# Loading each expert matrix of a mixture-of-experts kernel in four transfers instead of one

## The chip, the cores and the metric

The kernel runs on one core of a Trainium2 chip. The metric is the device time of one execution in microseconds (us), lower is better.

## The reference

Three layers run one after the other, all in float32:

```python
def reference(**kwargs):
    attn_out = _attn_ref(q, k, v)                      # 4 x 8 heads x 576 x 64, causal window of 64
    x = attn_out.transpose(0, 2, 1, 3).reshape(2304, 512)
    x = _moe_ref(x=x, w_skip, w_gate, w1, w2)
    return _moe2_ref(x=x, w_in, w_out)                 # 512 -> 2048, hard swish, 2048 -> 512

def _moe_ref(x, w_skip, w_gate, w1, w2):
    out = x.copy()
    xc = x[x @ w_skip > 0]
    logits = xc @ w_gate
    e_idx = np.argmax(logits, axis=1)
    for e in range(8):
        mask = e_idx == e
        h = np.maximum(xc[mask] @ w1[e], 0.0)          # w1[e]: 512 x 1024, 2 MB
        y[mask] = gate_w[mask, None] * (h @ w2[e])     # w2[e]: 1024 x 512, 2 MB
    out[do_compute] = xc + y
    return out
```

About half of the 2304 tokens are skipped; each of the others goes through one of eight experts.

## The kernel before

The instruction streams of the engines are written by hand and ordered by semaphores. There are three stages.

**Attention and routing** (to about 120 us). Eighteen blocks of 128 tokens are loaded, scored, and scattered by GpSimd (L696) to rows of a DRAM table, `x_rows`, so that the tokens of an expert stand together.

**Experts** (about 120 to 273 us). The tokens of each expert are worked on in tiles of 64; the number of tiles of an expert is read from a table at run time, so each engine has one hardware loop per expert. In this execution there are 17 tiles for the eight experts. For one tile TensorE makes the first product from `w1s` (L994, 128 matmuls), turns the tokens of the next tile around (L965, two transposes of `xin`), and makes the second product from `w2s` (L1006, 32 matmuls). ScalarE applies the relu, two chunks of the hidden layer at a time, to `hT` (L1245, four instructions for a tile), and copies the turned tokens to `xeT` (L1210). L1006 begins only when the first of the four `hT` instructions of its tile is done. VectorE forms the output `yo` (L1700), and GpSimd stores it to `x_rows` (L758). SyncE loads the tokens of a later tile to `xin`, in two transfers of 65 KB (L541), as soon as the two transposes of the one before have freed `xin`.

**Last layer** (about 273 us to the end). Six blocks at a time go through the 512 to 2048 to 512 layer (L1035, L1093), with weights that SyncE loads in small pieces (L548, L550, L556).

**The expert matrices.** There are three pairs of buffers, `w1s[e % 3]` and `w2s[e % 3]`, each with a semaphore of its own. The helpers `load_w1` (L321) and `load_w2` (L324) issue one transfer of 2 MB each, and `wait_w1` (L328) and `wait_w2` (L332) are TensorE's waits, the first at the head of an expert's loop, the second ahead of L1006 in each tile. SyncE loads expert 0 after the attention loads (L535), and expert 2 (L586) between the tiles of experts 0 and 1. ScalarE loads expert 1 after the first tile, and then, at the end of expert e, expert e + 3 into the pair that has come free (L1270, L1271), before it enters the loop of expert e + 1:

```python
                if e + 3 < NE:
                    sc.wait_ge(s_y, end)
                    fixed(sc)
                    load_w1(sc, e + 3, s_wp1[e % 3])
                    load_w2(sc, e + 3, s_wp2[e % 3])
```

Here `s_y` says that the last L1006 of expert e is done. ScalarE issues its own transfers in its own stream, so while it issues one it applies no relu. Below, "crossing e" is the time from the end of the last L1006 of expert e to the first L1006 of expert e + 1. Five crossings carry a load: those after experts 0 to 4.

Of the kernel before, what the change touches and what calls it, by code (L numbers as in the profile page):

```python
# [5 lines left out]
def attention_moe_mlp_kernel(nc, q, k, v, moe_w_skip, moe_w_gate, moe_w1, moe_w2,  # L6
# [20 lines left out]
    P = 128  # L27
# [10 lines left out]
    DC = DM // P  # L38
    FC = F // P
# [21 lines left out]
    with ctx:  # L61
# [3 lines left out]
        def sem(name):  # L65
            return ctx.enter_context(nc.semaphore(name))
# [19 lines left out]
        w1s, w2s = [], []  # L86
# [168 lines left out]
        s_wp1 = [sem(f"s_wp1_{i}") for i in range(3)]  # L255
        s_wp2 = [sem(f"s_wp2_{i}") for i in range(3)]
# [45 lines left out]
        SEQ = [LEAD] + list(range(LEAD)) + list(range(LEAD + 1, NE))  # L302
# [15 lines left out]
            eng.sem_inc(s_step, 1)  # L318

        def load_w1(eng, e, signal):  # L320
            eng.dma_start(w1s[e % 3][:, :, :], moe_w1[SEQ[e]].rearrange("(c p) f -> p c f", p=P)).then_inc(signal, 16)  # L321

        def load_w2(eng, e, signal):
            eng.dma_start(w2s[e % 3][:, :, :], moe_w2[SEQ[e]].rearrange("(c p) f -> p c f", p=P)).then_inc(signal, 16)  # L324

        def wait_w1(eng, e):

            eng.wait_ge(s_wp1[e % 3], 16 * (e // 3 + 1))  # L328

        def wait_w2(eng, e):  # L330

            eng.wait_ge(s_wp2[e % 3], 16 * (e // 3 + 1))  # L332

        def lg_bank(T):

# [174 lines left out]
        def _(sp):  # L510
# [20 lines left out]
            for T in range(1, NT):  # L531
                for n in loads_of(T):
                    load_qk(n)
                load_v(T)
            load_w1(sp, 0, s_wp1[0])  # L535
            load_w2(sp, 0, s_wp2[0])

            def load_rows(row):
# [35 lines left out]
            for e, first, end in expert_tiles(sp, first_bounds(sp)):  # L574
                base = R0 + e * R
                if e == 0:
                    with sp.Fori(0, end - 1) as t:
                        sp.wait_ge(s_ready, t + later + 1)
                        fixed(sp)
                        sp.wait_ge(s_xet, t + 1 + XT0)  # L580
                        sp.wait_ge(s_xmid, t + 1 + XM0)
                        load_rows(bass.ds(t * ET + (base + ET), ET))
                    continue
                if e == 1:
                    sp.wait_ge(s_ready, 2 * RD0)
                    load_w1(sp, 2, s_wp1[2])  # L586
                    load_w2(sp, 2, s_wp2[2])
                elif e == 2:
                    sp.wait_ge(s_padp, 16 * (NE - 2))
                elif e == 4:  # L590
                    load_w_in(0)
                elif e == 5:
                    load_w_out(0)
                    load_w_in(1)
                elif e == 7:
                    load_w_out(1)
                with sp.Fori(0, end - first) as t:
                    g = first + t
                    row = t * ET + base
                    sp.wait_ge(s_xet, g + XT0)  # L600
                    sp.wait_ge(s_xmid, g + XM0)
                    load_rows(bass.ds(row, ET))
# [174 lines left out]
        def _(pe):  # L777
# [203 lines left out]
            for e, first, end in expert_tiles(pe, bounds):  # L981
                wait_w1(pe, e)
                fixed(pe)
                with pe.Fori(0, end - first) as t:
                    g = first + t
                    pe.wait_ge(s_xetc, g + 1)
                    for m in range(FC // 2):

                        pe.wait_ge(s_hc, g * (FC // 2) + m - 4 + HC0 + 1)
                        for f in range(2 * m, 2 * m + 2):  # L990
                            for c in range(DC):
                                for x in range(2):
                                    cols = f * P + x * W
                                    last = pe.matmul(bank[m % 4][x * W:(x + 1) * W, (f % 2) * ET:(f % 2 + 1) * ET],  # L994
                                                     w1s[e % 3][:, c, cols:cols + W],
                                                     xeT[:, c % 2, c // 2, :], start=(c == 0), stop=(c == DC - 1))
                        last.then_inc(s_h, 1)
                    pe.wait_ge(s_xin, g * 32 + 64)
                    transpose_x()
                    wait_w2(pe, e)  # L1000
                    pe.wait_ge(s_yc, g + YC0)
                    for f in range(FC):
                        if f % 2 == 0:
                            pe.wait_ge(s_hc, g * (FC // 2) + f // 2 + HC0 + 1)
                        for x in range(2):
                            last = pe.matmul(bank[6][x * ET:(x + 1) * ET, 0:DH], hT[:, f, :],  # L1006
                                             w2s[e % 3][:, f, x * DH:(x + 1) * DH],
                                             start=(f == 0), stop=(f == FC - 1))
                    last.then_inc(s_y, 1)
# [115 lines left out]
        def _(sc):  # L1125
# [124 lines left out]
            for e, first, end in expert_tiles(sc, bounds):  # L1250
                if e == 0:
                    tile_of_expert(0)
                    sc.wait_ge(s_xin, 32 * 3)
                    load_w1(sc, 1, s_wp1[1])
                    load_w2(sc, 1, s_wp2[1])
                    first = 1
                with sc.Fori(0, end - first) as t:
                    tile_of_expert(first + t)
                if e == 4:
                    w_high(0)  # L1260
                    w_rest_high(0)
                elif e == 5:
                    o_high(0)
                elif e == 6:
                    w_high(1)
                    w_rest_high(1)
# [5 lines that stand above are left out]
# [605 lines left out]
```

## Time and profile before

| | |
|---|---|
| median of 3 runs | 666.27 us (664.95 to 668.8) |
| span of the profiled execution | 667.5 us |
| time of the profiled execution around its span | not listed; the span alone is |
| TensorE busy | 632.4 us, 95% of the span |
| ScalarE busy | 321.5 us, 48% |
| mean granted TensorE clock | 0.990 |
| bytes read and written in DRAM | 80.08 MB and 12.97 MB |
| the expert matrices among them | 16 transfers of 2048 KB |

The profile covers one execution. Its page gives the busy time of each engine and the chain of work that ended last. The chain is followed back from the last instruction: at each step it names what released the step. The timeline lists instructions by start and duration; issuing a transfer shows as a piece on the queue of its engine (SPq, ACTq), and the time to landing is counted from that issue to the last semaphore update.

### The profile page before, as it was taken

The page shows a single profiled execution, that of the slowest core. Times are in us where ns is not written, and L with a number is a line of the kernel's source. Part 1 is how long each engine was busy: PE and PEld are TensorE (multiplying, and loading weights), DVE is VectorE, ACT ScalarE, POOL GpSimd, SP SyncE. Part 2 cuts the span into 40 slices and gives each one's busy share as a digit, 9 for nine tenths or more (in the row PEclk, how much of TensorE's full clock was granted, in tenths as well). Part 3 has the DMA queues.
Part 4 walks back from the last instruction along what each step waited for, and adds up shares of the span by engine and source line. Part 5 has one row for each costly group of instructions (what it writes and reads, how often), then busy time and mean ns, then how long its engine had stood idle before and what let it go on. Part 6 is the DMA issues. An engine that isn't in the chain of part 4 may idle for free.

```text
span 667.5 us, 17127 instructions
## 1 busy us (share of the span) xinstructions
PE 632.4 (95%) x6454; PEld 549.9 (82%) x6454; DVE 396.2 (59%) x1070; ACT 321.5 (48%) x674; POOL 91.6 (14%) x160
## 2 busy tenths in 40 slices
PE   7899986798799989999999999999999999999998
PEld 6688874676678868898898898888888988888896
DVE  2678886311111122497766679777777788777743
ACT  3798884111112122664454556654455475444433
POOL 4333452431101011100000002100000021000000
PEclk9999999799989999999999999999999999999999
DMA  9876848498878785622222222623222233122102
GB/s 157 179 175 151 204 125 329 135 326 282 274 288 307 241 313 186 198 64 80 79 80 64 63 64 66 205 79 80 80 63 64 64 110 111 64 63 64 33 0 95
DMA packets 114132, 93.56 MB, mean 140 GB/s; under 512 B 62893, under 2 KB 90033, under 8 KB 114065
## 3 DMA queue, kind: packets, MB, share of 16 engines
q1 hardware_dynamic: 97696, 56.10, 30.9%
q10 hardware_dynamic: 12720, 25.58, 11.0%
q0 software_dynamic: 3648, 11.00, 4.4%
q8 instruction: 41, 0.67, 0.4%
q14 instruction: 27, 0.21, 0.1%
HBM read 80.08 MB, written 12.97 MB: 139 GB/s over the span
## 4 chain that ended last, share of the span: by engine, by line
PE 84%; DMA 4%; DVE 4%; issue 3%; ACT 1%; POOLq 1%; another core or an unknown queue 1%; POOL 0%; SPq 0%; DVEq 0%
PE bank L1093 30%; PE av L1035 27%; PE bank L994 7%; PE av L1006 7%; DMA xin<-x_rows 3%; PE bank L807 2%; PE av L851 2%; PE bank L792 2%; PE bank L867 2%; DVE sm L1460 1%; DMA x_rows<-yo,yrow 1%; PE av L965 1%; PE bank L897 1%; PE av L1022 1%
## 5 line engine op out<-in xcount | busy, mean ns | idle before, releaser
L1093 PE MATMUL bank<-o_hi,g_lo 128*128 128x512 f32 x288 | 114.0, 396 | 0.0
L1093 PE MATMUL bank<-o_hi,g_hi 128*128 128x512 f32 x288 | 113.9, 395 | 0.0
L1093 PE MATMUL bank<-o_lo,g_hi 128*128 128x512 f32 x288 | 113.5, 394 | 0.0
L1035 PE MATMUL av<-xc_hi,w_hi 128*128 128x384 f32 x344 | 89.5, 341 | 0.0
L1035 PE MATMUL av<-xc_hi,w_lo 128*128 128x384 f32 x344 | 88.3, 337 | 0.0
L1035 PE MATMUL av<-xc_lo,w_hi 128*128 128x384 f32 x344 | 88.2, 337 | 0.0
L1764 DVE TENSOR_TENSOR g_lo<-act,g_hi 128x384 fp32r<-128x384 f32 x96 | 53.4, 556 | 43.6 <-ACT g_hi L1328 40.4
L994 PEld LDWEIGHTS bank<-xeT,w1s 128*64 128x64 f32 x2176 | 69.2, 139 | 10.7 <-issue 8.4
L994 PE MATMUL bank<-xeT,w1s 128*64 128x64 f32 x2176 | 71.1, 224 | 6.4 <-issue 5.9
L1328 ACT CAST g_hi<-act 128x384 fp32r<-128x384 f32 x96 | 49.4, 515 | 51.4 <-DVE act L1757 49.4
L1035 PEld LDWEIGHTS av<-xc_hi,w_hi 128*128 128x128 f32 x344 | 63.0, 188 | 13.2 <-DVE act L1757 0.9
L1245 ACT ACTIVATE hT<-bank 128x128 f32<-128x128 f32 x68 | 18.8, 278 | 114.4 <-PE bank L994 108.4
L1318 ACT ACTIVATE rel<-hq,half 128x384 f32<-128x384 f32 x60 | 37.0, 617 | 70.4 <-DVE hq L1750 70.4
L1093 PEld LDWEIGHTS bank<-o_hi,g_lo 128*128 128x128 f32 x288 | 54.0, 188 | 13.0
L1006 PE MATMUL av<-w2s,hT 128*64 128x256 f32 x544 | 63.2, 385 | 0.3 <-DVE yo L1700 0.3
L1035 PEld LDWEIGHTS av<-xc_lo,w_hi 128*128 128x128 f32 x344 | 62.6, 188 | 0.0
L1035 PEld LDWEIGHTS av<-xc_hi,w_lo 128*128 128x128 f32 x344 | 62.4, 188 | 0.0
L1093 PEld LDWEIGHTS bank<-o_lo,g_hi 128*128 128x128 f32 x288 | 54.3, 188 | 6.5
L1093 PEld LDWEIGHTS bank<-o_hi,g_hi 128*128 128x128 f32 x288 | 54.0, 188 | 6.2
L1006 PEld LDWEIGHTS av<-w2s,hT 128*64 128x64 f32 x544 | 38.0, 138 | 20.8 <-issue 3.1
L1694 DVE COPY yo<-xres 128x4 f32<-128x4 f32 x17 | 2.9, 170 | 74.2 <-DMA x_rows<-yo,yrow 70.3
L1138 ACT ACTIVATE pr<-sm,mx 128x128 f32<-128x128 f32 x144 | 45.7, 396 | 1.4 <-DVE mx L1460 1.2
(182 smaller groups left out, 945.0 us busy)
## 6 DMA issues: line engine op xcount, KB each, us to landing
w1s<-in_moe_w ACTq DMA_DIRECT2D x6, 2048.0 KB, 10.1
w2s<-in_moe_w ACTq DMA_DIRECT2D x6, 2048.0 KB, 17.1
wor<-in_moe_w_out SPq DMA_DIRECT2D x24, 512.0 KB, 3.8
wir<-in_moe_w_in SPq DMA_DIRECT2D x24, 256.0 KB, 4.2
wir<-in_moe_w_in SPq DMA_DIRECT2D x48, 128.0 KB, 4.1
qraw<-in_q SPq DMA_DIRECT2D x36, 128.0 KB
vnow<-in_v SPq DMA_DIRECT2D x36, 128.0 KB, 3.6
kraw<-in_k SPq DMA_DIRECT2D x34, 128.0 KB
```

The source lines that it names most:

```text
L792: last = pe.transpose(dst[:, pi * P:(pi + 1) * P], src[:, 2 * pi:2 * pi + 2, :].rearrange("p h d -> p (h d)"), ident[:, :])
L807: last = pe.matmul(bank[2 + p][x * W:(x + 1) * W, j * KH:(j + 1) * KH], qT[T % 3][rows, j, x * W:(x + 1) * W], kT[T % 3][rows, j, 0:3:2, : ...
L851: last = pe.matmul(av[x * W:(x + 1) * W, h // HP, at0:at0 + VW], prT[T % 2][:, h, x * W:(x + 1) * W], (vnow if x else vprev)[:, T % 3, h, ...
L994: last = pe.matmul(bank[m % 4][x * W:(x + 1) * W, (f % 2) * ET:(f % 2 + 1) * ET], w1s[e % 3][:, c, cols:cols + W], xeT[:, c % 2, c // 2, : ...
L1006: last = pe.matmul(bank[6][x * ET:(x + 1) * ET, 0:DH], hT[:, f, :], w2s[e % 3][:, f, x * DH:(x + 1) * DH], start=(f == 0), stop=(f == FC - 1))
L1035: last = pe.matmul(into[:, 0:GN], a[it % 2][:, W_AT[w], c, :], b[:, X_AT[x], c, :], start=(n == 0 and fresh), stop=(n == 3 * XQ * len(pair ...
L1093: last = pe.matmul(bank[tile][:, :], a[c][:, i * P:(i + 1) * P], b[it % 2][:, units(it)[c], :], start=(p == 0 and c in (0, 2) and n == 0), ...
L1138: last = sc.activation(pr[T % 2][:, h, :], sm[:, h, :], ACT.Exp, scale=-1.0, bias=mx[T % 2][:, h:h + 1])
L1245: sc.activation(hT[:, 2 * m:2 * m + 2, :], bank[m % 4][:, 0:2 * ET].rearrange("p (f s) -> p f s", f=2), ACT.Relu).then_inc(s_hc, 1)
L1318: sc.activation(rel[n % 2][:, :], quarter(it, c), ACT.Relu, scale=1.0 / 6.0, bias=half[:, :]).then_inc(s_rel, 1)
L1328: sc.copy(g_hi[c][:, :], act[n % 2][:, :]).then_inc(s_ghi, 1)
L1764: dve.tensor_tensor(g_lo[c][:, :], act[n % 2][:, :], g_hi[c][:, :].bitcast(fp32), ALU.subtract).then_inc(s_glo, 1)
```

## The change

`load_w1` issues four transfers, one for each 128 rows of the matrix, and `load_w2` four, one for each two chunks of 128 rows. All four add to the semaphore that the one transfer added to, and the two waits ask for four times the count. Where the loads stand in the streams, the buffers and the bytes are as before.

```diff
         def load_w1(eng, e, signal):
-            eng.dma_start(w1s[e % 3][:, :, :], moe_w1[SEQ[e]].rearrange("(c p) f -> p c f", p=P)).then_inc(signal, 16)
+            for c in range(DC):
+                eng.dma_start(w1s[e % 3][:, c, :], moe_w1[SEQ[e], c * P:(c + 1) * P, :]).then_inc(signal, 16)
 
         def load_w2(eng, e, signal):
-            eng.dma_start(w2s[e % 3][:, :, :], moe_w2[SEQ[e]].rearrange("(c p) f -> p c f", p=P)).then_inc(signal, 16)
+            rows = moe_w2[SEQ[e]].rearrange("(c p) f -> p c f", p=P)
+            for c in range(0, FC, 2):
+                eng.dma_start(w2s[e % 3][:, c:c + 2, :], rows[:, c:c + 2, :]).then_inc(signal, 16)
 
         def wait_w1(eng, e):
 
-            eng.wait_ge(s_wp1[e % 3], 16 * (e // 3 + 1))
+            eng.wait_ge(s_wp1[e % 3], 16 * DC * (e // 3 + 1))
 
         def wait_w2(eng, e):
 
-            eng.wait_ge(s_wp2[e % 3], 16 * (e // 3 + 1))
+            eng.wait_ge(s_wp2[e % 3], 16 * (FC // 2) * (e // 3 + 1))
```

Here DC is 4 and FC is 8.

## Rows read from the trace of the kernel before

**Rows 1.** The page: its head, and the chain that ended last, by engine.

```profile
span 667.5 us, 17127 instructions
PE 84%; DMA 4%; DVE 4%; issue 3%; ACT 1%; POOLq 1%; another core or an unknown queue 1%; POOL 0%; SPq 0%; DVEq 0%
```

**Rows 2.** The chain in order of time, expert stage (start us, us, what).

```profile
155.91 9.37 DMA xin<-x_rows
...
165.76 3.60 PE av L1006 x32
...
173.92 3.60 PE av L1006 x32
...
180.20 3.42 issue
...
186.12 4.32 PE av L1006 x32
...
198.46 2.67 PE bank L994 x91
...
203.01 3.60 PE av L1006 x32
...
226.85 0.38 PE av L965 x2
...
228.10 7.72 DMA xin<-x_rows
...
264.83 2.73 PE bank L994 x93
```

**Rows 3.** Issue to landing of the 2 MB transfers, L321 and then L324.

```profile
DMA to landing us min/median/max: 8.8/10.1/14.1
...
DMA to landing us min/median/max: 14.5/17.0/20.0
```

**Rows 4.** Timeline of ScalarE at crossings (start us, us, engine line op out<-in).

```profile
169.92 1.09 ACTq L324 DMA_DIRECT2D w2s<-in_moe_w  x1
171.75 0.28 ACT L1245 ACTIVATE hT<-bank 128x128 f32<-128x128 f32 x1 [5.58 <-issue]
...
178.06 0.75 ACTq L324 DMA_DIRECT2D w2s<-in_moe_w  x1
...
198.59 0.37 ACTq L321 DMA_DIRECT2D w1s<-in_moe_w  x1
198.99 0.53 ACTq L324 DMA_DIRECT2D w2s<-in_moe_w  x1
200.29 0.28 ACT L1245 ACTIVATE hT<-bank 128x128 f32<-128x128 f32 x1 [5.02 <-PE bank L994]
...
224.57 0.28 ACT L1245 ACTIVATE hT<-bank 128x128 f32<-128x128 f32 x1 [5.12 <-PE bank L994]
```

**Rows 5.** Lines L556 and L635: what issuing one takes (ns min/median/max).

```profile
L556 SPq DMA_DIRECT2D wor<-in_moe_w_out x24: 367/368/506, 221.2 to 616.8; - x24
...
L635 SPq DMA_DIRECT2D out<-ot x3: 332/351/360, 661.4 to 662.8; - x3
```

**Rows 6.** Timeline of SyncE: the load of expert 2, and a run of small loads.

```profile
150.40 0.51 SPq L324 DMA_DIRECT2D w2s<-in_moe_w  x1
155.24 11.87 SPq L541 DMA_DIRECT2D xin<-x_rows  x4
...
262.52 1.44 SPq L616 DMA_DIRECT2D xn<-x_rows  x3
264.01 1.39 SPq L616 DMA_DIRECT2D x_first<-x_rows  x3
...
267.93 0.51 SPq L556 DMA_DIRECT2D wor<-in_moe_w_out  x1
```

**Rows 7.** Issue to landing of `wor` (512 KB), and of `x_first` (260 KB each).

```profile
DMA to landing us min/median/max: 3.6/3.8/8.3
...
DMA to landing us min/median/max: 5.4/5.5/5.7
```

## The prediction, made before the kernel was run

> **What bounds the kernel now.** I read the page first, then the chain in order of time, then the timeline of the two engines that issue the loads. TensorE carries 84% of the chain that ended last, DMA 4% and "issue" 3% [rows 1]. The change touches the transfers of the expert stage alone, so the question is where that stage has a gap that a weight load makes. The chain shows three large ones [rows 2]. From 155.91 it waits 9.37 us for `xin`. That transfer was issued on SyncE's queue behind the 4 MB of expert 2, issued there to 150.91 [rows 6]. From 228.10 it waits 7.72 us for `xin` again, while the matrices of expert 6 are in flight, though these are on ScalarE's queue; most of that lies beside TensorE's work: a tile takes 8.16 us from L1006 to L1006 (165.76 to 173.92), so after the L1006 of 227.23 the next was due at 235.4, and it began after 235.82 + 0.44 = 236.3. And from 180.20 TensorE stands 3.42 us in the middle of the first tile of expert 2 with nothing it waited for ("issue"). The L1006 after it takes 4.32 us instead of 3.60.
>
> No gap is a wait for the matrices themselves. A load is issued almost two experts ahead. The shortest cover is expert 7: its `w2` is issued by about 241, the slowest of the six took 20.0 us to land [rows 3], so 261, and its first L994 begins at 264.83 [rows 2]. So nothing is gained by matrices that arrive sooner, and the new waits ask for all four pieces anyway.
>
> **The change, part by part.**
>
> *Waits with four times the count.* The same number of instructions, and they are satisfied when the last piece is in, as before. Nothing; the cover is the 3.8 us just worked out for expert 7. If the eight pieces took over 3.8 us longer, that expert would wait.
>
> *Issue on SyncE, experts 0 and 2.* Two issues become eight. For one quarter of `w2` there is a row with the same shape, 2 x 128 pieces of 2 KB: `wor`, 0.37 us, 0.51 at most. For a quarter of `w1` (128 contiguous rows) the nearest is `out`, 0.33 to 0.36 us [rows 5]; I take 0.36. With 0.03 us between two issues, eight take 4 x 0.39 + 4 x 0.40 = 3.2 us, against 0.38 + 0.03 + 0.51 = 0.92 us. So SyncE comes free 2.2 us later. For expert 2 that is 153.2 instead of 150.9. What is queued behind is the load of `xin`, which does not go out before 155.24 [rows 6], since `xin` is not free sooner. Hidden, with 2 us to spare. For expert 0 SyncE has nothing else to issue for about ten microseconds.
>
> *Issue on ScalarE, experts 1 and 3 to 7.* This is the term that can show. Expert 1 is loaded early in a tile, with the relus all behind it and over 4 us of TensorE's L994 ahead of the L1006 that needs them: hidden. At the five crossings the budget is tighter. At crossing 2, L1006 ends at 198.46; ScalarE issues `w1` from 198.59, `w2` to 199.52, spends 0.77 us on entering the next loop, and runs its first `hT` at 200.29, done at 200.57. TensorE asks for that `hT` at 203.01 [rows 2, 4]. The slack is 2.44 us and the added issue time 2.2 us: hidden, by 0.2 us. Crossing 3: `hT` done at 224.85, asked for at 226.85 + 0.38 = 227.23, slack 2.38: hidden, by 0.2 us. Crossing 0: the `w2` issue took 1.09 us there, `hT` was done at 172.03, asked for at 173.92, slack 1.89: 0.3 us late. Crossing 1: the 3.42 us stop puts the next L1006 at 186.12, so all is hidden. Crossing 4 has the same steps as crossing 2. The three later `hT` come 0.3 us apart and are asked for every 0.9 us, so only the first counts. Sum: +0.3 us, say +0.4 with the signal. Lower bound 0. Upper bound: all eight cost what the dearest similar issue did, 0.51 to 0.53 us plus 0.03, so 4.5 us, 3.5 more than before: 1.6 late at crossing 0, and 1.1 at each of 2, 3 and 4, or 4.9 us in all.
>
> *The transfers themselves.* The bytes, the row sizes and the engine that moves them are unchanged; only the order of rows within `w1` differs, and each piece ends with a completion of its own, six more per expert. No row has a piece boundary alone. The nearest is the run of three `xn` and three `x_first` from 262.52: the last is issued at about 264.97 and landed 5.7 us later, so six loads of 260 KB took 8.15 us [rows 6, 7]. The same 1.56 MB at the rate of a 2 MB load that follows another (2 MB in the 17.0 - 10.1 = 6.9 us between the landings of `w1` and `w2` [rows 3]) is 5.2 us, plus 1.3 us at the start as an estimate from 3.8 us for the 512 KB of `wor` (1.7 us of data, the rest split between start and completion). That leaves 1.65 us for five boundaries, 0.3 each at most, and other traffic ran beside it. Six more boundaries are at most 2.0 us per expert. Hidden wherever the matrices have cover; on the path once, at expert 2, since `xin` waits behind them (9.37 us). I take 0, since the pieces follow in one queue without a wait. Bounds: below, -1 us, should contiguous rows of `w1` be read faster; above, +2.0 us.
>
> The sum against the profiled execution is 667.5 + 0.4 = 667.9 us. Its span is 1.2 us above the median of the runs, so on the median: 666.3 + 0.4 = **666.7 us**. A measurement of this kernel can tell about 0.5%, 3.3 us, from no change.
>
> **The rivals.**
>
> *A. The issues hold ScalarE (slower).* An issue may wait when many transfers are outstanding on its queue. For it: 0.75 us at 178.06, while the load of expert 3 was still in flight, against 0.53 us [rows 4]. Against it: at 267.93 SyncE issued `wor` in 0.51 us with three `x_first` (landing 5.5 us after 264 to 265) and three `wir` outstanding, six in all [rows 6, 7]. With eight issues, the eighth has seven ahead of it, and at crossing 1 eleven. It decides from the point where the first `hT` is done later than 4.55 us after the last L1006. If the eighth has to wait for the first piece to land (3.8 us, as `wor`), ScalarE is free at 4.3, `hT` done at 5.3 us: 0.8 us late at four crossings; at crossing 1, where it would have to wait for expert 3 to land at about 187, some 2 us after the stop. With the tail of such waits, +3 to +8 us: 669 to 674 us, 672 as its middle.
>
> *B. Each piece pays its own start and end (slower).* If pieces went one after another, each would take the 3.8 us of `wor`: 30 us instead of the 17.4 for the pair, 13 us more, on the path at `xin` behind expert 2, and about 5 us at expert 7, past its cover: 666.3 + 13 + 5 = 684 us. Against it: the six loads above, 1.36 us each where a lone 512 KB takes 3.8.
> The Trainium skill (DMA: Bandwidth & Descriptors, "Anatomy of one DMA" and "Rules for kernel authors") puts a fixed cost of some 2.0 us on one DMA (stated for GpSimd's path) and asks for 1 MiB or more in each. Six more of these per expert would be 12 us if they added up; the trace of six loads in 8.15 us speaks against their adding up.
>
> *C. Small transfers get their turn sooner (faster).* If what stops TensorE at 180.20, and `xin` at 228.10, is waiting behind long runs of a big transfer, shorter ones may let them in sooner. All of it would be 3.42 + 0.72 us and about 1 us, some 5 us: 661.5 us; a share of it is likelier. Against it: the pieces stand in the queue one right behind the other, as the one transfer did.
>
> *D. The change does not do what it says.* Issues in the trace are counted per transfer, so four per matrix will show; nothing merges them. I give it nothing of its own.
>
> **How the numbers follow.** Forecast (hidden, but for tenths) 0.74; A 0.13; B 0.04; C 0.09. The forecast's own range is 664.5 to 669.5. The range for all, with the bounds of the ScalarE term (+4.9) and half of A, is 663.5 to 671.5. Faster by over 0.5% (below 663.0): half of C and a little of run to run change, 0.07. Slower by over 0.5% (above 669.6): B, most of A, and the upper end of the issue term, 0.17. Within 0.5%: 0.76.
>
> **What would show it.** In the profile of the changed kernel: 24 issues of `w1s` and 24 of `w2s` on ACTq of 512 KB each, 0.35 to 0.40 us apiece; the first `hT` after a crossing some 4.0 us after the end of L1006, not 1.8; L1006 to L1006 over a crossing unchanged at 8.15 us or up by a few tenths. SyncE's `xin` after expert 2 still issued near 155.2 and landing near 165.3. `w1s` complete at about 10 us and `w2s` at about 17 us after the first issue. It is wrong if an issue on ACTq takes over 0.6 us in the median (A), if `xin` after expert 2 lands several us later (B), or if the stop at 180.20 is gone (C).

## The result, and the profile after

The changed kernel takes 676.4 us (median of 4 runs, 674.33 to 679.82), against 666.46 us for the kernel before. The ratio is 1.0138, with a 95% interval of 1.0095 to 1.0181: 1.4% slower. The profiled execution took 674.66 us; its span is 673.0 us, 5.5 us above that of the profile before. It is one of the two quicker runs of the four, and the profile before is that of the slowest run of its kernel (668.8 us), so the two profiles show about half of the loss.

The page of the changed kernel, its head and the chain that ended last:

```profile
span 673.0 us, 17175 instructions
PE 86%; DVE 4%; ACTq 3%; issue 2%; DMA 2%; ACT 2%; another core or an unknown queue 1%; SPq 0%; DVEq 0%
```

ACTq, ScalarE's issuing of transfers, is on the chain now with 3%; before it had no share at all [rows 1]. DMA went down from 4% to 2%. So the chain does not wait for transfers to move, but for an engine to issue them. The chain in order of time, at crossing 2 (start us, us, what; L1009 is the L1006 of before, L997 the L994, L1248 the L1245):

```profile
195.35 3.63 PE av L1009 x32
...
199.08 0.35 ACTq L322
...
199.46 0.46 ACTq L322
...
199.94 0.46 ACTq L322
...
200.43 0.62 ACTq L322
...
201.08 0.48 ACTq L327
...
201.59 0.54 ACTq L327
...
202.16 1.49 ACTq L327
...
203.68 0.73 ACTq L327
...
205.18 0.29 ACT hT L1248
...
205.51 1.08 PE av L1009 x7
```

From L1009 to L1009 it is 10.16 us here; before it was 8.15 us (194.86 in the trace of before, to 203.01 [rows 2]). The eight issues took 5.33 us, from 199.08 to 204.41, where the prediction had put 3.2 us. Their durations over the whole kernel (ns min/median/max):

```profile
L322 ACTq DMA_DIRECT2D w1s<-in_moe_w x24: 352/455/1431, 133.8 to 246.6; - x24
L322 SPq DMA_DIRECT2D w1s<-in_moe_w x8: 348/434/621, 95.9 to 151.0; - x8
...
L327 ACTq DMA_DIRECT2D w2s<-in_moe_w x24: 455/573/1575, 135.6 to 248.7; - x24
L327 SPq DMA_DIRECT2D w2s<-in_moe_w x8: 469/662/846, 98.0 to 153.7; - x8
```

The piece of `w2` has the shape of `wor`, which took 367/368/506 ns [rows 5], and the median here is 573 ns on ScalarE. Only the first issue of `w1` in a run takes 0.35 to 0.38 us; those right behind it take 0.45 us and more.

The waits of the expert stage (engine, line, waited for: us in total, times, longest):

```profile
PEld av L1009 <- ACT hT L1248: 7.9, 5, 2.3
...
PE av L1009 <- ACT hT L1248: 6.6, 4, 2.0
```

TensorE waits 6.6 us for `hT`, four times; before, only the weight load showed such a wait, 0.9 us in total. From the L1006 at the start of crossing 0 to the last one it was 103.58 us before (165.76 to 269.34) and is 109.45 us now (165.43 to 274.88), 5.9 us more. By the same starts the crossings 0 to 4 took 8.16, 12.20, 8.15, 8.19 and 8.75 us before and 10.14, 11.58, 10.16, 9.92 and 8.97 us now: 5.3 us more. Crossing 1 hides it in this run, since there an "issue" stop stood in both kernels, 3.42 us before and 1.92 us now.

At the other four the prediction's own sum, filled with what was measured, gives the loss (us; the time held runs from the start of the first issue to the end of the last):

| crossing | held before | held now | added | slack before | added less slack | crossing longer by |
|---|---|---|---|---|---|---|
| 0 | 1.51 | 5.33 | 3.82 | 1.89 | 1.93 | 1.98 |
| 2 | 0.93 | 5.33 | 4.40 | 2.44 | 1.96 | 2.01 |
| 3 | 1.03 | 5.09 | 4.06 | 2.38 | 1.68 | 1.73 |
| 4 | 0.94 | 4.15 | 3.21 | 3.03 | 0.18 | 0.22 |

The load of expert 2 on SyncE cost nothing here: its eight issues ran from 149.66 to 154.22, 4.56 us, and `xin` behind them was issued at 155.03. It is waited for from 155.90 for 9.06 us; before it was 155.91 and 9.37 us [rows 2].

### The profile page after: what moved, and what is told of

Same layout as the page of the kernel before. It is cut to its first block, busy times and chain, and to the rows that moved or that the text cites. A ratio compares the mean times of both kernels' runs of the same rounds, so it can differ in the third digit from the quotient of the medians.

```text
span 673.0 us, 17175 instructions
## 1 busy us (share of the span) xinstructions
PE 635.3 (94%) x6454; PEld 551.0 (82%) x6454; DVE 396.2 (59%) x1070; ACT 319.6 (47%) x674; POOL 91.1 (14%) x160
## 4 chain that ended last, share of the span: by engine, by line
PE 86%; DVE 4%; ACTq 3%; issue 2%; DMA 2%; ACT 2%; another core or an unknown queue 1%; SPq 0%; DVEq 0%
PE bank L1096 30%; PE av L1038 27%; PE av L1009 9%; PE bank L997 7%; PE bank L810 2%; PE av L854 2%; PE bank L795 2%; PE bank L870 2%; ACTq L327 2%; DVE sm L1463 1%; DMA xin<-x_rows 1%; ACTq L322 1%; PE av L968 1%; PE bank L900 1%
## 5 line engine op out<-in xcount | busy, mean ns | idle before, releaser
L997 PEld LDWEIGHTS bank<-xeT,w1s 128*64 128x64 f32 x2176 | 69.8, 140 | 9.5 <-issue 7.2
L997 PE MATMUL bank<-xeT,w1s 128*64 128x64 f32 x2176 | 72.2, 225 | 4.7 <-issue 4.0
L1248 ACT ACTIVATE hT<-bank 128x128 f32<-128x128 f32 x68 | 17.2, 279 | 123.7 <-PE bank L997 95.3
L1009 PE MATMUL av<-w2s,hT 128*64 128x256 f32 x544 | 64.3, 390 | 7.1 <-ACT hT L1248 6.6
L1009 PEld LDWEIGHTS av<-w2s,hT 128*64 128x64 f32 x544 | 38.4, 140 | 28.6 <-ACT hT L1248 7.9
```

The lines of the kernel that those rows point to most:

```text
L1248: sc.activation(hT[:, 2 * m:2 * m + 2, :], bank[m % 4][:, 0:2 * ET].rearrange("p (f s) -> p f s", f=2), ACT.Relu).then_inc(s_hc, 1)
```

## The experiments

The runs were made on several chips, on which the kernel before takes 652 to 668 us, so each is compared with runs of the kernel before on the same chip. Lines are numbered anew in each kernel.

**1. Which engine's pieces cost.** Only ScalarE's loads cut in four:

```diff
+        def parts1(e):
+            return 1 if e in (0, 2) else 4
```

> Only the loads that ScalarE issues (experts 1 and 3 to 7) are cut in four; SyncE's two (experts 0 and 2) are one transfer of 2 MB each again. Theory I (the extra issues hold ScalarE at the crossings): as slow as the changed kernel, 8 to 11 us above before. Rival T (the small pieces slow the transfers, and what waits behind them): the xin behind expert 2 is as before, so part of the loss comes back, by 2 us or more.

Measured: 670.08 against 652.69 us, ratio 1.0262 (1.0194 to 1.033). The loss is there, and it is larger than the 1.4% of the first chip; the changed kernel itself did not run on this one. In the profile TensorE's matmuls wait 10.8 us for `hT`, in place of 6.6, and two of the second products (the L1006 of before) behind such waits, at 229.74 and 248.62, take 5.07 and 5.36 us in place of 3.60. The slack is smaller on this chip too: with ScalarE's loads whole (the next run) crossings 0, 2 and 3 take 7.7 us from L1006 to L1006, against 8.15 to 8.19 us on the first chip.

Only SyncE's loads cut in four (`return 4 if e in (0, 2) else 1`):

> Only SyncE's loads (experts 0 and 2) are cut in four. Theory I: as before, within 1.5 us, since SyncE has time to spare. Rival T: slower by 2 us or more, with xin landing after 165.8 us in the chain where before it landed at 165.3.

Measured: 656.49 against 652.69 us, ratio 1.0035 (0.9992 to 1.0079), not to be told from no change, though 5 us is not excluded: in its profile the chain runs through SyncE's eight issues (141.38 to 146.09) to the `xin` behind them. Most of the loss, at the least, lies where ScalarE issues the pieces.

**2. Issues without the pieces.** The matrices whole, and six tiny transfers behind them at each crossing:

```diff
                     load_w2(sc, e + 3, s_wp2[e % 3])
+                    for n in range(6 * e, 6 * e + 6):
+                        sc.dma_start(lgs[n // 15][:, n % 15 * 8:n % 15 * 8 + 8], moe_w2[0, 0:P, n * 8:n * 8 + 8]).then_inc(s_tiny, 16)
```

> The matrices are loaded in transfers of 2 MB as before, and at each of the five crossings ScalarE issues six more transfers of 4 KB in all (128 rows of 32 bytes) to a tile that nothing reads. Theory I: slower by 5 to 11 us, like the changed kernel, with the first relu after a crossing 5 to 6 us after the last L1006 in place of 2. Rival T: within 1.5 us of before, as the big transfers are whole.

Measured: 698.74 against 652.69 us, ratio 1.0717 (1.0639 to 1.0795). The sign was right, and the loss of 46 us over four times the largest that was expected. The issues (ns min/median/max), and ScalarE's timeline at crossing 1:

```profile
L1275 ACTq DMA_DIRECT2D lgs<-in_moe_w x30: 505/772/6447, 162.9 to 270.3; - x30
```

```profile
177.29 0.39 ACTq L322 DMA_DIRECT2D w1s<-in_moe_w  x1
177.71 0.53 ACTq L325 DMA_DIRECT2D w2s<-in_moe_w  x1
178.27 9.21 ACTq L1275 DMA_DIRECT2D lgs<-in_moe_w  x6
```

Six transfers of 4 KB take 9.21 us to issue, and the first of them alone, right behind the two of 2 MB, took 4.88 us; at the five crossings the first took 3.9 to 6.4 us. So what an issue costs is not a constant: here the first transfer behind 4 MB just issued blocked its engine for microseconds each time. In the changed kernel the last of the eight has 3.5 MB ahead of it. This run therefore shows more than the changed kernel holds, and can't stand for it.

**3. The hold without any transfer.** The matrices whole, and ten chained copies on ScalarE at each crossing:

```diff
                     load_w2(sc, e + 3, s_wp2[e % 3])
+                    for n in range(10 * e, 10 * e + 10):
+                        sc.copy(lgs[1][:, :], lgs[0][:, :]).then_inc(s_tiny, 1)
+                        sc.wait_ge(s_tiny, n + 1)
```

> Transfers of 2 MB as before, and no more of them; at each of the five crossings ScalarE makes ten chained copies of 128 x 128, of no use to the result, some 3 to 4 us in all, between its loads and the relus. Theory I (it is the time that ScalarE is held, whatever holds it): as slow as the changed kernel, 8 to 18 us. Rival T (the transfers): as before, within 1.5 us.

Measured: 673.37 against 666.39 us, ratio 1.0107 (1.0049 to 1.0165), and for the changed kernel in the same set of runs:

> The changed kernel, unchanged, on the chip of these runs. Theory I: slower by 10 to 18 us, of it 8 us or more at the crossings from L1006 to L1006. Rival T: the loss lies at the first tiles, where xin waits behind expert 2.

Measured: 675.19 against 666.39 us, ratio 1.0121 (1.0081 to 1.0161). Both losses are a little under what had been expected. ScalarE's timeline of the copies at crossing 2, and TensorE's waits for `hT` in that run (L1007 is the L1006 of before):

```profile
199.20 0.53 ACTq L325 DMA_DIRECT2D w2s<-in_moe_w  x1
199.77 3.27 ACT L1274 COPY lgs<-lgs 128x128 f32<-128x128 f32 x10 [4.30 <-issue]
204.12 0.79 ACT L1246 ACTIVATE hT<-bank 128x128 f32<-128x128 f32 x4 [1.07 <-issue]
```

```profile
PE av L1007 <- ACT hT L1246: 4.9, 5, 1.2
```

3.3 us of work between the loads and the relus, with every transfer as before, make the kernel slower by 7 us by the ratios, where the changed kernel lost 8. The intervals are wide, 3 to 11 us for the copies, so the share of seven eighths is not exact. TensorE waits less in the profile with the copies, 4.9 us against 9.5 in that of the changed kernel on this chip, as the shorter hold would have it. That a hold of ScalarE alone slows the kernel by this much is shown, and no property of the smaller transfers is needed for it.

The profiled run of the changed kernel here was its slowest, 679.6 us, and shows what the milder profile above did not. Its chain (start us, us, what):

```profile
177.31 3.70 PE av L1009 x32
...
181.48 1.67 ACTq L322
...
185.73 1.91 ACTq L327
...
188.71 5.36 PE av L1009 x32
...
198.56 3.63 PE av L1009 x32
...
208.57 5.36 PE av L1009 x32
...
226.46 3.63 PE av L1009 x32
...
236.79 5.36 PE av L1009 x32
```

The kernel before, once more, on the same chip:

> The kernel before, unchanged, for a profile on the chip of these runs. A crossing with a load takes about 8 us from L1006 to L1006 (7.7 without one), and the first relu after the issues starts 1.8 to 2.0 us after the last L1006.

It took 664.21 us. Its chain:

```profile
165.46 5.29 PE av L1006 x32
...
175.32 3.60 PE av L1006 x32
...
184.31 6.84 DMA xin<-x_rows
...
191.63 3.60 PE av L1006 x32
...
199.80 3.60 PE av L1006 x32
...
215.96 3.60 PE av L1006 x32
224.11 3.60 PE av L1006 x32
```

Crossings 2 and 3 take 8.17 and 8.15 us there, and 10.01 and 10.33 us in the changed kernel. Crossing 1, without a stop in either kernel, takes 8.1 and 11.4 us: ScalarE was held 6.54 us there in place of 1.02, with a slack of 2.3 us.

And three L1009 that follow a late `hT` take 5.36 us in place of 3.60. The granted clock of two of them, of the middle of the first, and of one that waited for nothing (stretch, us, busy us of PE, PEld, DVE, ACT and POOL with their counts, PEclk, DMA share, GB/s):

```profile
188.71:194.07 5.36, 5.36 (x38) 3.28 (x40) 0.00 (x0) 0.72 (x4) 0.00 (x0) 0.68 1.03 366
189.10:192.30 3.20, 3.20 (x18) 1.72 (x16) 0.00 (x0) 0.33 (x2) 0.00 (x0) 0.50 1.04 356
208.57:213.93 5.36, 5.36 (x38) 3.29 (x40) 0.29 (x2) 0.83 (x4) 0.00 (x0) 0.68 1.05 374
218.43:222.03 3.60, 3.60 (x38) 2.46 (x40) 0.29 (x2) 0.37 (x1) 0.00 (x0) 1.00 0.16 43
```

After these waits the granted clock is down from 2.4 to 1.2 GHz (0.50) for part of the product, and that costs 1.76 us more. Not every such wait is followed by it. In the profile of 674.66 us the L1009 at 205.51 had waited about 2 us too and ran at the full clock:

```profile
205.51:209.18 3.67, 3.67 (x38) 2.53 (x40) 0.29 (x2) 0.82 (x4) 0.00 (x0) 1.00 1.01 374
```

Nor is it the changed kernel's alone: the L1006 of 5.29 us at 165.46 above, behind the wait for `xin`, ran at 0.68 in the kernel before. An L1009 of 5.36 us stands once in the profile of 674.66 us (at 231.63) and three times in the one of 679.6 us: two more are 3.5 of the 4.9 us between them. Against the kernel before on this chip, from the L1006 at the start of crossing 0 to the last one it was 99.03 us (165.46 to 264.49) and is 113.88 us (166.01 to 279.89), 14.9 us more: about 9 in the five crossings and 5.3 in these three L1009. The two are the fastest run of one kernel and the slowest of the other, so this adds up an extreme case, not the median.

**4. How many pieces fit.** Two transfers of 1 MB for each matrix; then only `w1`, and only `w2`, in four:

> Each matrix in two transfers of 1 MB. ScalarE is held 0.95 to 1.1 us more at each crossing, under the slack of about 2.4 us there. Theory I: as before, within 2 us. A rival by which each further transfer costs in proportion, whatever the slack: a third of the loss of the changed kernel, 3 to 4 us.

> w1 in four transfers of 512 KB, w2 in one. ScalarE is held some 1.5 us more at each crossing (three more issues of 0.46 + 0.03 us), up to 2.5 us where an issue is stretched by 1 us. Theory I: within 2 us of before. Proportional rival: 4 to 5 us slower.

> w2 in four transfers of 512 KB, w1 in one. ScalarE is held 1.8 us more at each crossing, 2.8 or more where an issue is stretched: past the slack there. Theory I: 1 to 4 us slower than before. Proportional rival: 4 to 6 us slower.

Measured, against 654.64 us: halves 653.34 us, ratio 0.9992 (0.9954 to 1.0031); `w1` only 658.19 us, 1.0027 (0.9988 to 1.0066); `w2` only 659.15 us, 1.0039 (0.9998 to 1.008). By the ratios two more issues cost nothing (-3 to +2 us) and three cost 2 to 3 us, neither of which is clear of zero; six cost 8 to 17 us on other chips. The halves contradict a loss in proportion, which would be 3 to 4 us, and agree with a slack that swallows the first 2 us. The two with three more issues do not decide: their upper ends, 4 and 5 us, reach what the proportional rival says. In the halves' profile one crossing was still late:

```profile
169.84 0.94 ACTq L330 DMA_DIRECT2D w1s<-in_moe_w  x2
170.81 3.56 ACTq L336 DMA_DIRECT2D w2s<-in_moe_w  x2
175.12 0.78 ACT L1257 ACTIVATE hT<-bank 128x128 f32<-128x128 f32 x4 [8.60 <-issue]
```

This is crossing 1, with expert 3 still in flight (issued from 162.15, and no `w2` transfer of this run landed in under 11.1 us): two issues take 3.56 us, the second of them 3.04. With `w2` alone in four it was the same crossing: 11.35 us from L1006 to L1006 against 7.70 where nothing waits, with a single issue of 2.55 us.

**5. The pieces kept, the hold moved.** The load of expert e + 3 stands behind the first tile of expert e + 1 (expert 1 has one tile in these inputs, so its loop is left out; the code would not do for all inputs):

```diff
+                elif e + 2 < NE:
+                    tile_of_expert(first)
+                    load_w1(sc, e + 2, s_wp1[(e + 2) % 3])
+                    load_w2(sc, e + 2, s_wp2[(e + 2) % 3])
+                    first = first + 1
```

First with four pieces:

> All matrices are cut in four, but ScalarE issues the load of expert e + 3 after the four relus and the xeT copy of the first tile of expert e + 1, some 5 us later, in place of ahead of them (for this the first tile stands ahead of the loop; expert 1 has one tile only). Theory I: the loss is gone, 0 to 3 us below before or within 1 us of it, and no wait of L1006 for hT of over 0.3 us at the crossings. Rival T: slower than before by 5 us or more still.

Measured: 663.22 against 652.69 us, ratio 1.0155 (1.0053 to 1.0257). That was a miss: the wait of TensorE's matmuls for `hT` was down to 0.7 us in its profile, but the time was not back. With transfers of 2 MB in the same place, on another chip:

> Transfers of 2 MB, issued behind the first tile of the next expert as in the late version with four. Theory I: the crossings are as before or 0.3 us shorter; the kernel is within 3 us of before. If the late version with four was slow because of where its loads lie beside xin, this one is slower than before by 4 us or more too, and its longest tiles are those with a load in their midst; if it was slow because of the pieces, this one is as before.

Measured: 671.39 against 666.39 us, ratio 1.0068 (1.0037 to 1.01), so on this chip the place costs something by itself. What the pieces add could not be read from two chips, so the pair ran again on one, beside a version with `w1` at the crossing and `w2` behind the tile:

> The late version with four transfers once more, beside the late version with one. If pieces cost nothing where ScalarE has the time, the two are within 0.4% of each other, both 0.3 to 1% slower than before (the later load lies beside xin). If they cost by themselves, this one is slower than the other by 0.7% or more.

> The late version with transfers of 2 MB once more, the partner of the run before: 0.3 to 1% slower than before.

> All matrices in four transfers as in the changed kernel, but ScalarE's hold is cut in two: the four issues of w1 stand at the crossing, the four of w2 behind the relus of the first tile after it. Each hold is some 2 to 3 us. Theory I: most of the loss is gone, within 3 us of before. If the pieces cost by themselves, wherever they are issued: as slow as the changed kernel, 8 us or more.

Measured, against 668.35 us: four pieces late 667.19 us, ratio 0.999 (0.9954 to 1.0025); whole late 668.66 us, 1.0012 (0.9983 to 1.0041); hold cut in two 665.91 us, 0.9974 (0.9938 to 1.001). The last has all 64 pieces and is as fast as the kernel before. Its waits at L1018, the L1006 of before, and its ScalarE at crossing 2:

```profile
PEld av L1018 <- ACT hT L1257: 0.3, 2, 0.2
```

```profile
198.18 1.99 ACTq L330 DMA_DIRECT2D w1s<-in_moe_w  x4
200.87 0.85 ACT L1257 ACTIVATE hT<-bank 128x128 f32<-128x128 f32 x3 [6.01 <-issue]
202.20 0.28 ACT L1257 ACTIVATE hT<-bank 128x128 f32<-128x128 f32 x1 [0.49 <-PE bank L1006]
202.57 0.37 ACT L1222 COPY xeT<-av 128x256 f32<-128x256 f32 x1
202.58 2.32 ACTq L336 DMA_DIRECT2D w2s<-in_moe_w  x4
```

Four issues take 1.99 us and end before the relus are due; the other four take 2.32 us where ScalarE waits for TensorE anyway. So the pieces cost nothing that can be seen where ScalarE is not held past its slack (-4 to +1 us by the interval). The two late versions were within 0.4% of each other, as expected, but not slower than before: neither repeated its earlier ratio on this chip. Why the first late version was 1.6% slower stays open. Its profile shows three things that the repeat's does not: a single issue of 3.14 us on the chain (at 182.76), and two L1018 of 4.89 and 4.81 us in place of 3.60 (at 212.78 and 240.26).

**6. The wait for `xin` at the first tiles.** Transfers of 2 MB; expert 2 is issued by ScalarE behind the second tile, not by SyncE ahead of `xin`:

> Transfers of 2 MB; the load of expert 2 is issued by ScalarE behind the relus of the second tile, some 10 us earlier than SyncE issued it, so that it no longer stands ahead of xin on SyncE's queue. If the wait of 9 to 10 us for xin at the first tiles is due to that queue, it shrinks to 4 to 7 us, and the kernel is 2 to 4 us faster than before; if it is due to the traffic as a whole, it is as before within 1.5 us.

Measured: 652.03 against 654.64 us, ratio 0.9951 (0.991 to 0.9993): 0.5% faster, about 3 us (0.5 to 6). This is a little better than the kernel before, and has nothing to do with the size of the transfers. In its profile the waits of the chain for `xin` are of 6.2 to 6.8 us, and none of 9 us is left. That the queue was the cause of the longer wait fits this; the kernel before has no profile from this chip. The price stands in the same profile: the `w2` load of expert 2, issued at 132.47 right behind its `w1` and 5 us behind the 4 MB of expert 1, held ScalarE for 5.64 us.

## Why the prediction was wrong

The forecast was 666.7 us in a range of 663.5 to 671.5; the time was 676.4 us. Slower by over 0.5% had been given 17%.

- *What bounds the kernel, the cover of the matrices, the waits with four times the count, SyncE's issues*: right in what they say of the time: no wait for a matrix appeared, and SyncE's pieces alone gave 1.0035 (0.9992 to 1.0079). SyncE's eight issues took 4.56 us all the same, not 3.2, and were hidden by 0.8 us, not by 2.
- *Issue on ScalarE*: the place and the mechanism were right, and the step that failed is the size of this term, "The slack is 2.44 us and the added issue time 2.2 us: hidden, by 0.2 us", which gave +0.4 us in all, with 4.9 us as its upper bound. The added time was 3.2 to 4.4 us at crossings 0, 2, 3 and 4, and 5.5 us at crossing 1 of the slowest run; the rest of the sum holds within 0.1 us, as the table shows. The eight issues were priced at 0.36 and 0.37 us from `out` and `wor`, the medians of rows where an issue mostly stands first or alone. The one `wor` of rows 6 that followed others, at 267.93, took 0.51 us. Behind one another they take 0.46 (`w1`) and 0.57 us (`w2`) in the median, and in each of the first four crossings loaded at least one took 1.0 to 1.6 us. ScalarE was held 5.33 us at crossing 2, not 3.2, and the first `hT` began 6.2 us after the end of L1009, not 4.0. The nearer row was in the forecast's own group: the three `x_first`, issued in a run, took 1.39 us with the spacing, 0.46 each [rows 6]. Eight at 0.47 would have been 3.8 us, past the slack at every crossing but the last, and the 1.09 us of `w2` [rows 4] was a sign that one in such a run gets stretched, not an accident of crossing 0.
- *A margin of 0.2 us treated as hidden.* The working found slack 2.4 us against 2.2 us added. A difference so near its limit is no zero: each further 0.1 us counts at every crossing. Crossing 1 was set to nothing because of the stop of 3.42 us; in later profiles that stop was absent (8.1 us in the later profile of the kernel before), and the changed kernel lost 3.3 us there. Crossing 4 did not have "the same steps as crossing 2": its slack was 3.03 us, and it lost 0.2 us.
- *What follows a late `hT`.* The forecast had noted 4.32 in place of 3.60 us after a stop, but gave such a stop no price of its own. Where the granted clock is down behind such a wait, one L1009 takes 1.76 us more: once in the milder profile, three times in the slowest. This was left out of the sum and of its upper bound.
- *The transfers themselves*: 0 fits what was found. The hold alone, by copies, gives 1.0107 beside 1.0121, and the pieces with the hold cut in two give 0.9974 (0.9938 to 1.001).
- *Rival A* named the sign, the engine and, at 672 with 669 to 674 us, nearly the size, with 13%. Its mechanism is partly borne out: issues do block behind a backlog (4.88 us behind 4 MB, 3.04 us at crossing 1 of the halves). But the eight issues of crossings 0, 2, 3 and 4 took 4.2 to 5.3 us with no single one over 1.49 us, and by the forecast's own sign for A, a median over 0.6 us, it was not A: the medians are 0.455 and 0.573. The evidence against it, `wor` with six small transfers outstanding, was about their number, and did not bear on megabytes in flight.
- *Rival B*: contradicted; `xin` behind expert 2 did not land later (its wait ended at 164.96, before at 165.28). The Trainium skill's rule in DMA: Bandwidth & Descriptors, "Rules for kernel authors", to use 1 MiB or more per DMA for the highest bandwidth, gives the better choice here, but the runs show another reason than a fixed time on the transfer: the time of the engine that issues it. The Trainium skill's page Perfetto Trace Analysis, "Optimizing DMA Performance", names that resource, the sequencer of the issuing engine, as one of the things that can bound a kernel. At a crossing the trace agrees, with ScalarE's queue issuing from 199.08 to 204.41; over the whole span ACTq is 3% of the chain, and TensorE bounds the kernel.
- *Rival C*: no gain in sight; the stop was 1.92 us in this profile and came and went in both kernels.

## What to carry to other kernels

Count an issue as time of the engine that makes it, and price a run of issues by rows where issues follow one another, with a longer one in most runs of eight. Where an engine both issues loads and does work that another waits for, put the issues where it waits anyway, or no more of them than the slack holds; here four transfers then cost no more than one. If the slack and the added time are within a few tenths of each other, forecast the loss, and give the fall of the clock that can follow the wait a price.

## What the runs showed of the hardware that was not expected

- A transfer of 4 KB issued right behind two of 2 MB held ScalarE for 3.9 to 6.4 us, and one of 2 MB, issued right behind another and 5 us behind two more, for 5.64 us (experiment 6). What limits it was not tried apart.
- An issue of 512 KB of `w1` takes 0.35 to 0.38 us when it is the first of a run and 0.46 us in most cases when it is the next, on ScalarE.
- In the changed kernel's trace the longest issues of crossings 0 to 3 (1.43, 1.58, 1.49 and 1.02 us) each overlap a 16 KB packet of the instruction queue in the trace's DMA records. That one causes the other was not tested, and the longest issue of the slowest run, 1.91 us, overlaps none.
